# The second network's output products in token form, two neighbouring places in one row: four places per chunk instead of eight

## The reference

```python
w = softmax(weight, axis=-1)                        # 8 heads x 7 taps
x1[s] = sum over k of w[head, k] * x[s - 6 + k]     # a causal mix over 7 tokens
y = (silu(x1 @ w_gate) * (x1 @ w_val)) @ w_out1     # 192 -> 1536 -> 192
h = y @ w_in2                                       # 192 -> 2048
out = where(h > 0, h, exp(min(h, 0)) - 1) @ w_out2  # 2048 -> 192
```

## Time and profile before

| | us |
|---|---|
| median of 3 runs (1181.9 to 1182.41) | 1181.98 |
| the profiled execution | 1181.17 |
| its span, first to last instruction | 1179.4 |
| one chunk in the loop (604.23 to 676.92, the same place) | 72.69 |
| TensorE matmul busy | 1174.7 |
| VectorE, ScalarE, GpSimd busy | 758.5, 666.5, 698.3 |

### The profile page before, as it was taken

How to read it: one execution, slowest core, us unless ns; L and a number is a source line. 1 busy time by engine, 2 the same in 40 slices (tenths; PEclk the granted TensorE clock), 3 DMA queues, 4 the chain that set the end, 5 groups by cost and what they waited for, 6 DMA issues and landing times.

```text
span 1179.4 us, 31411 instructions
## 1 busy us (share of the span) xinstructions
PE 1174.7 (100%) x11804; PEld 1032.3 (88%) x11804; DVE 758.5 (64%) x1193; ACT 666.5 (57%) x1114; POOL 698.3 (59%) x517
## 2 busy tenths in 40 slices
PE   9999999999999999999999999999999999999999
PEld 8999889898888988889888898888988889888898
DVE  7877565675646766566664766647566475675665
ACT  6557555464554646546465564655646556465565
POOL 6378566474654746557465474655757456475565
PEclk9999999999999999999999999999999999999999
DMA  7512011121111211012110021200212002120110
GB/s 176 119 52 46 12 35 34 32 44 28 25 23 31 44 31 27 18 31 44 31 36 14 26 44 31 41 12 22 44 31 44 9 22 44 31 44 9 32 33 15
DMA packets 103956, 43.38 MB, mean 37 GB/s; under 512 B 75888, under 2 KB 93936, under 8 KB 103920
## 3 DMA queue, kind: packets, MB, share of 16 engines
q1 hardware_dynamic: 103104, 42.29, 16.1%
q10 hardware_dynamic: 816, 0.59, 0.2%
HBM read 16.12 MB, written 6.29 MB: 19 GB/s over the span
## 4 chain that ended last, share of the span: by engine, by line
PE 100%; ACT 0%; DVE 0%; issue 0%
PE up L904 56%; PE down L904 44%; PE down L1118 0%; ACT in_a_hi L652 0%; DVE stage L743 0%; ACT stage L672 0%; DVE halos L828 0%
## 5 line engine op out<-in xcount | busy, mean ns | idle before, releaser
L450 POOL TENSOR_TENSOR hid_lo<-hidden,hid_hi 128x512 fp32r<-128x512 f32 x435 | 598.8, 1389 | 454.5 <-ACT hid_hi L589 296.2
L904 PE MATMUL down<-out_w,hid_hi 64*128 64x384 f32 x2040 | 297.6, 353 | 0.0
L765 DVE TENSOR_TENSOR hidden<-act,up 128x512 f32<-128x512 f32 x191 | 130.8, 685 | 236.0 <-ACT act L572 236.0
L904 PE MATMUL down<-out_w,hid_lo 64*128 64x192 f32 x2040 | 256.4, 247 | 0.0
L806 DVE TENSOR_SCALAR act<-up 128x512 f32<-128x512 f32 x256 | 164.7, 685 | 124.3 <-PE up L904 122.5
L904 PE MATMUL up<-in_b_hi,up_w_hi 64*128 64x512 f32 x1128 | 222.1, 388 | 0.0
L589 ACT ACTIVATE hid_hi<-hidden 128x512 fp32r<-128x512 f32 x192 | 121.5, 633 | 176.4 <-DVE hidden L765 158.4
L904 PE MATMUL up<-in_b_hi,up_w_lo 64*128 64x512 f32 x1128 | 221.1, 387 | 0.0
L904 PE MATMUL up<-in_b_lo,up_w_hi 64*128 64x512 f32 x1128 | 221.0, 386 | 0.0
L608 ACT ACTIVATE act<-act 128x512 f32<-128x512 f32 x256 | 157.1, 632 | 102.0 <-DVE act L806 102.0
L904 PEld LDWEIGHTS down<-out_w,hid_lo 64*128 64x128 f32 x2040 | 195.2, 187 | 4.9
(11 more groups left out here) (99 smaller groups left out, 1083.6 us busy)
## 6 DMA issues: line engine op xcount, KB each, us to landing
x_raw<-x_dram SPq DMA_DIRECT2D x136, 64.0 KB, 2.2
out_dram<-stage SPq DMA_DIRECT2D x15, 384.0 KB, 2.7
in_b_hi<-in_b_hi SPq DMA_DIRECT2D x32, 128.0 KB, 2.3
in_b_lo<-in_b_lo SPq DMA_DIRECT2D x32, 128.0 KB, 2.3
swapped<-halves SPq DMA_DIRECT2D x32, 128.0 KB, 2.3
in_a_hi<-in_a_hi SPq DMA_DIRECT2D x30, 128.0 KB, 2.3
in_a_lo<-in_a_lo SPq DMA_DIRECT2D x30, 128.0 KB, 2.3
stage<-w_out_dram SPq DMA_DIRECT2D x7, 384.0 KB, 4.5
```

What stands on the lines that cost most here:

```text
L450: return pool.tensor_tensor(hid_lo[:, slot, :], hidden[:, s, :], hid_hi[:, slot, :].bitcast(F32), ALU.subtract)
L765: v.tensor_tensor(hidden[:, f % 2, :], act[:, f % 2, :], val_bank(f, n)[:, :], ALU.mult)\
L904: return nc.tensor.matmul(dst, lhsT, rhs, start=start, stop=stop, skip_group_check=True)
```

## The change

A pair no longer stands behind every step. In `elu_phase` two pairs stand behind j = 3, 5 and 7 (the pairs 0 and 2, 4 and 6, 8 and 10), nothing behind j = 2, 4 and 6. The pairs 12 and 14 both stand behind f = 1 of the next `mix_phase`, nothing of the second network behind f = 0. No matmul is added or removed, and no other engine's code is changed. `elu_phase(16)` had the pairs 12 and 14 of chunk 14 together behind its step j = 0 already.

```diff
-                    if f < 2 and is_int(n, 2) and N2 - LAG2 + 2 * f in OUT2_AT:
-                        wait_weights(pe, OUT2_AT[N2 - LAG2 + 2 * f])
-                    if f < 2 and not (chunk0 or chunk1):
-                        down2_pair(n - 2, N2 - LAG2 + 2 * f)
+                    if f == 1 and not (chunk0 or chunk1):
+                        if is_int(n, 2):
+                            wait_weights(pe, len(pieces))
+                        for k in range(N2 - LAG2, N2, 2):
+                            down2_pair(n - 2, k)
...
-                    if j >= 2:
-                        if is_int(n, 1) and 2 * j - LAG2 in OUT2_AT:
-                            wait_weights(pe, OUT2_AT[2 * j - LAG2])
-                        down2_pair(n - 1, 2 * j - LAG2)
+                    if j >= 3 and j % 2:
+                        for k in (2 * j - LAG2 - 2, 2 * j - LAG2):
+                            if is_int(n, 1) and k in OUT2_AT:
+                                wait_weights(pe, OUT2_AT[k])
+                            down2_pair(n - 1, k)
```

## The result

| | before | after |
|---|---|---|
| median | 1181.98 us (1181.5 to 1182.41, 5 runs) | 1213.53 us (1212.64 to 1213.71, 5 runs) |
| ratio, 95% interval | | 1.027 [1.026, 1.0281] |
| profiled execution, its span | 1181.17, 1179.4 | 1213.6, 1211.9 |
| one chunk in the loop, mean of 12 rounds | 72.69 | 74.65 |

The change costs 31.6 us, 2.7%. 34.6 were forecast. The rounds are counted from the start of the projection j = 1 in chunk 1 to the same place 12 chunks on: (1036.31 - 163.99) / 12 before, (1062.78 - 166.95) / 12 after.

What follows compares the result with a forecast made beforehand. TensorE (PE) was taken as the bound, waiting for nobody after 13 us. Terms -0.6 + 16.8 + 6.2 + 11.3 + 0.9 = +34.6 us on the profiled 1181.17 gave 1215.8, as median 1216.5 us, 2.9% slower; range 1196 to 1226.

Steps and rivals of the forecast that it cites:

- j = 3, 16 phases: Projection j = 3, without pair 0 before it, waits for the activations of k = 2 and 3: 16.8 us.
- 31 places that the ring's chain just reaches: At j = 5, f = 1 and the last j = 7, only a start of 0.20 us each is lost: 6.2 us.
- j = 7 with in1_lo, 15 phases: VectorE's in1_lo meets POOL's low parts, adding 0.55 to the start's 0.20 us at j = 7: 11.3 us.
- the end: Pairs 8, 10, 12 follow one another; pair 12 waits inside for the low part of k = 13: 0.9 us.
- 62 merges: Putting two single pairs into a double one saves 0.01 us each through fewer alternations with projections: -0.6 us.
- The chain behind a first pair: High part, POOL's low parts, then activation after a double pair's first pair; ends just when the next projection would start.
- E + 4.32: Forecast end of that activation, in us after E, when PE goes on from a double pair's first pair.
- the price of a start: Time PE loses starting again after a wait: taken as 0.20 us, between 0.14 and 0.23.
- rival (2): POOL runs both low parts before in1_lo gets in, adding 9 us: 1225 us; chance 0.10.
- Rival (1): Only j = 3 waits; the second chain and in1_lo cost nothing: +17.1 us, 1199; chance 0.20.
- What kept its cover: Waits at f = 2 and f = 3, POOL's sums, `fold_y_tail` and the next chunk's input stay covered: costed at nothing.

Runs made afterwards that it cites:

- experiment 6: Changed kernel with pair 0 back behind j = 2, pair 2 behind j = 3, and six ring places for the second network: 1182.16 us, ratio 1.001.
- experiment 7: Kernel before with one double pair, 12 and 14 together behind f = 1, nothing behind f = 0: 1181.93 us, ratio 1.0006.
- experiment 1: Kernel before with one double pair: nothing behind j = 2, pairs 0 and 2 behind j = 3: 1198.42 us, ratio 1.014.
- experiment 4: Changed kernel with six places instead of four in the second network's rings of high and low parts: 1198.89 us, ratio 1.015.
- experiment 3: Changed kernel with VectorE's first in1_lo (in2_lo in phase 15) behind the two activations of j = 5 instead of before them: 1205.39 us, ratio 1.0206.
- experiment 2: Changed kernel with pair 0 put back behind j = 2 and pair 2 alone behind j = 3: 1193.33 us, ratio 1.0103.
- experiment 5: Kernel before with double pairs behind j = 4, j = 6 and f = 0, pair 0 behind j = 2, 14 behind f = 1: 1200.92 us, ratio 1.0164.

## Why the prediction was right

The measured 1213.5 lies 3.0 us under the forecast, and the mechanism was the one described. That the sum came so near is in part luck: two terms were 5.6 us too large together, one was 1.8 too small, and 1.3 us of the difference between the two profiled executions are in no term. Point by point, in us over the whole kernel:

| term | forecast | measured | from |
|---|---|---|---|
| j = 3, 16 phases | 16.8 | 16.9 | 15 times 7.14 to 7.21 and once 7.45 against 6.12 |
| 31 places that the ring's chain just reaches | 6.2 | 3.3 | 4.22 to 4.28 against 4.15 |
| j = 7 with in1_lo, 15 phases | 11.3 | 8.6 | 4.71 to 4.75 against 4.15 |
| the end | 0.9 | 0.9 | below |
| 62 merges | -0.6 | +1.2 | periods of experiments 6 and 7 |
| sum | 34.6 | 30.9 | |

- **The wait of j = 3** came out to 0.1 us. The chain from the mins to the activations was read as rigid, and it is: it ends 0.82 us after j = 2 here too (619.78 against 618.96). Experiments 1 and 4 leave nothing but it.
- **The chain behind a first pair** was put at E + 4.32 and is E + 4.29. It was rightly found to end just when PE is due. What was too large is the price of a start, 0.20 for each: where PE hardly waits, a start costs 0.11, of which the slow first matmuls are 0.09. Forecast bounds were 0.05 to 0.25.
- **in1_lo at j = 7** was put at 0.55 and is 0.46. It goes between POOL's two low parts, as the earlier trace rows had it, so rival (2), in which POOL keeps its turn, is out. Rival (1), in which only j = 3 costs anything, is out with the two rows above it in the table. In the trace in1_lo starts at 634.55 and ends at 635.92, 0.55 behind the end of POOL's first low part (634.07 + 1.30 = 635.37). The Trainium skill, "SBUF — State Buffer", section Who interferes with whom, says that the one that issues second is blocked in full. The trace agrees to about 0.1 us, as in1_lo takes 0.68 alone. Who is next it does not say; here VectorE got in between. The same change of places freed `fold_y_tail` of such a meeting: it takes 1.28 in the changed kernel where it took 1.83 in the loop before, on nobody's path.
- **The end.** Pair 12 waits inside, for the low part of k = 13, as forecast:

```profile
1203.41 0.36 PE L904 MATMUL down<-out_w,hid_hi 64*128 64x384 f32 x2
1204.41 0.36 PE L904 MATMUL down<-out_w,hid_lo 64*128 64x192 f32 x2 [0.64 <-POOL hid_lo L450]
1204.60 0.36 PE L904 MATMUL down<-out_w,hid_hi 64*128 64x384 f32 x2
```

  1.00 between the first two where 0.20 is usual, and 0.19 between the next two where it is 0.09: 0.9.
- **The merges** are the step that was wrong, in its sign. I took it that one longer projection follows a double pair as it follows a single one. But of the one double pair that the trace before had, I read only the front; the next row of that kind was there:

```profile
1147.71 0.33 PE L904 MATMUL down<-out_w,hid_hi 64*128 64x384 f32 x2
```

  From 1143.57 to it are 4.14 us for two projections, not 2.04 + 2.08 = 4.12. A double pair and its two projections take 4.53 + 4.15 = 8.68, two single ones with theirs 2 x (2.25 + 2.08) = 8.66. The periods say it sharper: 72.69 us grow to 72.71 with one merge in a chunk and to 72.75 with three, 0.02 for each. So with these waits taken away the merges still bring nothing.
- **What kept its cover** did: no wait shows at f = 2, f = 3, or in the rest of the mix phase.

The sum of the terms is 30.9, the medians differ by 31.6, the two profiled executions by 32.4. In the latter, 0.8 us lie before the two kernels do anything different, in front of the first chunk's end (PE reaches this row at 53.10 us before):

```profile
53.91 0.39 PE L904 MATMUL up<-in_b_hi,up_w_hi 64*128 64x512 f32 x2
```

They are not the change's: over the ten profiled executions the start of j = 1 in the first second-network phase lies anywhere between 89.64 and 92.13 us (91.18 before, 91.99 after, 91.22 in experiment 3). Another 0.5 are 7 of the 62 double pairs, five behind j = 3 and two behind j = 7, that take 4.60 to 4.61 instead of 4.53. The matmuls go a little slower there, and nothing is waited for. The same is seen in two double pairs of experiment 2, one of experiment 3 and three of experiment 5, and in none of the others; the cause stays open.

## What to carry to other kernels

When work is moved away from between a wait and its release, take both numbers from the trace, the end of the chain and the moment at which the bound engine now arrives; an engine that is busy all the time says nothing about how far its releases were ahead. Follow each resource that a moved instruction frees, too: a ring of as many places as one batch takes leaves no reserve. Two more places removed 46 of 62 waits here, and gave nothing in the kernel before, where nobody waited for the ring. And measure the gain that is hoped for at both of its edges before the costs: a row at the front and one at the back of the one double pair would have shown that there was none.

## What the runs showed of the hardware

- **A start costs even where the matmul's row names no wait.** When the release came 0.07 us before the matmul was due (628.60, 628.67), PE shows no idle time, but the first two matmuls took 0.32 us instead of 0.23 until the next. With the release earlier (experiment 4) the same two projections took 4.15 instead of 4.22 to 4.28. The short waits stand in the list of the weight loads, which has all 62, where that of the matmuls has 31.
- **VectorE got in between two queued operations of POOL.** Both were TENSOR_TENSOR with two operands in SBUF: 3.00 us for two low parts, against 2.54 to 2.56 alone, and 1.36 or 1.37 for the VectorE operation against 0.68, in each of 15 phases.
- **Fewer changes between the two forms of matmul gained nothing.** Both are of 64 rows, with 512 columns moving or 384 and 192; grouping them by twos cost 0.02 us for each group.
